# Moving the attention's keys and values by 64 bytes in a partition

## The reference

```python
scores = scale * np.matmul(q, k.transpose(0, 1, 3, 2))      # q, k, v: 4 x 8 heads x 576 x 64
scores = np.where(masks, scores, -1e9)                      # heads 0-3 local (32 back), 4-7 strided by 32
attn = softmax(scores)
x = (attn @ v), heads side by side                          # 2304 tokens x 512
h = x @ w_in; x = (h * sigmoid(1.702 * h)) @ w_out          # dense FFN, 512 -> 2048 -> 512
# then: tokens with x @ w_skip > 0 go to one of 8 experts (argmax of x @ w_gate),
# y = relu(x @ w1[e]) @ w2[e] (512 -> 1024 -> 512), out = x + gate * y; the others stay x
```

## The kernel before

| tile | bytes | address before | behind a multiple of 128 | of 256 |
|---|---|---|---|---|
| w_hi, w_lo, ident, gate_w | | 16512, 82048, 155776, 156800 | 0 | 128 |
| qs0, qs1 | 2304 | 165568, 167872 | 64 | 192 |
| ks0, ks1 | 2304 | 170176, 172480 | 64 | 192 |
| vs0, vs1 | 3072 | 174784, 177856 | 64 | 192 |
| probs0 to probs3 | 1536 | 180928 ... 185536 | 64 | 192 |
| probsT0, probsT1 | 1536 | 187456, 188992 | 64 | 64 |
| x_stage, x_hi, x_lo, g_hi, g_lo, x2, x2T | | 190528 and on | 64 | 64 |
| expert tiles read by TensorE (xg, xe, relu_h, h_hi, h_lo, h_rest) | | 164160 and on | 64 | 64 |

## Time and profile before

### The profile page before, as it was taken

The page is one execution under the profiler, slowest core; times in us unless marked ns, Lnnn a source line. Parts: engine busy times, 40 slices in busy tenths (PEclk is TensorE's granted clock), DMA queues, the critical chain, the costliest instruction groups (busy, mean ns, idle before and its releaser), DMA issues.

```text
span 700.0 us, 12990 instructions
## 1 busy us (share of the span) xinstructions
PE 654.6 (94%) x4457; PEld 560.1 (80%) x4458; DVE 392.2 (56%) x1374; ACT 356.4 (51%) x1025; POOL 156.1 (22%) x172
## 2 busy tenths in 40 slices
PE   3779999999999999999999999999998899998893
PEld 3568888888888889989899899898886687876772
DVE  4867774555445534334243343344658876878762
ACT  4878766655655533333333333334445665565650
POOL 5335421231223102001010010010114553213431
PEclk9989999999999999999999999999999999999897
DMA  7637634333421250201102002003346766577620
GB/s 243 202 126 249 216 105 161 100 95 109 132 74 40 79 168 1 91 1 31 61 1 90 0 0 90 0 1 106 91 136 179 251 223 214 178 250 246 212 93 14
DMA packets 45154, 81.53 MB, mean 116 GB/s; under 512 B 6594, under 2 KB 10690, under 8 KB 45088
## 3 DMA queue, kind: packets, MB, share of 16 engines
q1 hardware_dynamic: 41360, 75.01, 32.7%
q0 software_dynamic: 3184, 4.64, 2.1%
q10 hardware_dynamic: 544, 1.05, 0.4%
HBM read 65.06 MB, written 17.47 MB: 118 GB/s over the span
## 4 chain that ended last, share of the span: by engine, by line
PE 80%; DVE 5%; POOL 5%; DMA 3%; issue 3%; ACT 3%; POOLq 0%; DVEq 0%; ACTq 0%
PE ph L1440 28%; PE px L1453 28%; PE py L1573 5%; PE pe_h L1541 3%; PE pscore L1390 3%; PE ptrans L1399 3%; PE pctx L1412 2%; PE py L1577 2%; PE pe_h L1545 2%; DMA w_raw<-we 1%; DVE w_lo L1012 1%; PE phT L1557 1%; PE ph L1464 1%; POOL probs L689 1%; POOL slot_table L697 1%
## 5 line engine op out<-in xcount | busy, mean ns | idle before, releaser
L1440 PE MATMUL ph<-x_hi,w_hi 128*128 128x256 f32 x576 | 166.1, 288 | 1.0 <-DVE x_lo L1073 1.0
L1168 DVE SCALAR_TENSOR_TENSOR gated<-gated,ph 128x256 f32<-128x256 f32 x144 | 60.6, 421 | 187.7 <-ACT gated L902 186.4
L1440 PE MATMUL ph<-x_lo,w_hi 128*128 128x256 f32 x576 | 160.5, 279 | 0.0
L1440 PE MATMUL ph<-x_hi,w_lo 128*128 128x256 f32 x576 | 160.3, 278 | 0.0
L1453 PE MATMUL px<-w_hi,g_hi 128*128 128x512 f32 x288 | 117.7, 409 | 0.0
L1440 PEld LDWEIGHTS ph<-x_hi,w_hi 128*128 128x128 f32 x576 | 108.4, 188 | 8.2 <-issue 3.3
L1453 PE MATMUL px<-w_hi,g_lo 128*128 128x512 f32 x288 | 113.6, 394 | 0.0
L1453 PE MATMUL px<-w_lo,g_hi 128*128 128x512 f32 x288 | 113.0, 392 | 0.0
L1440 PEld LDWEIGHTS ph<-x_lo,w_hi 128*128 128x128 f32 x576 | 108.8, 189 | 3.6
L1440 PEld LDWEIGHTS ph<-x_hi,w_lo 128*128 128x128 f32 x576 | 108.7, 189 | 0.0
L902 ACT ACTIVATE gated<-ph 128x256 f32<-128x256 f32 x144 | 54.9, 381 | 102.3 <-PE ph L1440 99.3
(11 more groups left out here) (215 smaller groups left out, 1041.4 us busy)
## 6 DMA issues: line engine op xcount, KB each, us to landing
w_raw<-we SPq DMA_DIRECT2D x64, 256.0 KB, 2.9
more_raw<-we SPq DMA_DIRECT2D x64, 256.0 KB, 3.8
w_raw<-wf SPq DMA_DIRECT2D x32, 256.0 KB, 3.8
vs<-vw SPq DMA_DIRECT2D x16, 384.0 KB, 3.5
qs<-qT SPq DMA_DIRECT2D x16, 288.0 KB, 3.9
ks<-kT SPq DMA_DIRECT2D x16, 288.0 KB, 4.4
xT_dram<-x_stage SPq DMA_DIRECT2D x16, 288.0 KB, 3.3
x_lo<-xT_dram SPq DMA_DIRECT2D x8, 512.0 KB, 3.6
```

What stands on the lines that cost most here:

```text
L1168: nc.vector.scalar_tensor_tensor(gated[s % 2][:, :], gated[s % 2][:, :], 1.0, ph[s % 2][:, 0:TT], ALU.add, ALU.mult).then_inc(gated_done, 1)
L1440: last = nc.tensor.matmul(ph[f % 2][:, 0:TT], up_w(w, k, f), x[p][:, k, :], start=(at == 0 and n == 0), stop=(at == KD - 1 and n == 2))
```

## The change

Two tiles that nothing reads or writes are allocated, 64 bytes a partition each (16 float32): one between the queries and the keys, one between the values and the probabilities. Keys and values then begin at multiples of 128 bytes (ks0 at 170240, vs0 at 174848), and everything allocated behind the values moves by 128 bytes. Queries, masks, weights and the expert tiles stay where they are. No instruction is added or moved.

```diff
         qs = [sb(f"qs{i}", [P, S], to=ffn) for i in range(2)]
+
+        sb("gap_before_keys", [P, 16], to=ffn)
         ks = [sb(f"ks{i}", [P, S], to=ffn) for i in range(2)]
         vs = [sb(f"vs{i}", [P, 2, MAXBLK, D], to=ffn) for i in range(2)]
+        sb("gap_behind_values", [P, 16], to=ffn)
         probs = [sb(f"probs{i}", [P, MAXU, P], to=ffn) for i in range(SLOTS)]
```

## The result

The changed kernel takes 710.69 us (median of 4 runs, 706.74 to 711.85), the kernel before 702.8 in the same comparison (700.56 to 705.01). The ratio is 1.0088 with a 95% interval of 1.0052 to 1.0123: slower by 0.9%. The time lies above the forecast range, which ended at 706.7.

The account below looks back on a forecast made before the run. TensorE's own instructions were taken as the bound from 48 us through the dense stages. Attention -0.2, dense matmuls 0 and DMAs 0 gave 701.4 us for the profiled execution, 703.1 for the median, range 699.5 to 706.7.

Parts of the forecast that it names:

- What bounds the kernel: From 48 to 245 us and in the dense stage behind, TensorE's own instructions bound the kernel; before 48 us it waits.
- Scores and context: Attention's fp32 matmuls in the TensorE-bound stage: the changed address halves give -0.2 us, with -1.2 and +1.8 as ends.
- DMAs: Writes of keys and values: any alignment effect on the first keys, -0.5 to 0 us, would be hidden; price 0.
- The dense matmuls: Up and down matmuls, beside and dense stages: sequence entry, not place, picks the pace; price 0 us.
- the exchange of signs: Dense up and down swap their opposite-signed operand differences modulo 256; both cost alike per column, so price 0.
- The second rival: TensorE settles in its slower dense pace in both stages, x and g 192 behind 256: 8.5 us, 711.8; chance 0.07.
- The sum against the median: Whole kernel: -0.2 us on the profiled 701.6 gives 701.4; the runs' median, 703.3, is 1.7 higher, so forecast 703.1.

Follow-up runs that it names:

- the grid: A kernel of its own, not computing the reference: TensorE alone runs dense and score-like matmuls at varied operand places; up takes 113.3 ns at distance 64, 117.8 at 192.

## Why the prediction was wrong

- **What bounds the kernel**: right. The change's price was read where it was said to be, in TensorE's own pieces, and the waits did not move.
- **Scores and context**, -0.2 us with -1.2 and +1.8 as ends: right, and the truth was nearer 0. The nearest row, the transposes with their halves apart, told it: 0.90 and 0.72 us a group before and after, and no pair of places in the grid changes the form.
- **DMAs**, 0: right. Keys land after 4.5 us for 4.4, and nobody waits.
- **The dense matmuls**, 0: this is the step that failed, and two sentences of it. First, "the same operands at the same addresses have both paces, so what picks one is how the sequence enters, not where a tile lies". The first half of it holds: the entry counts, at either place. But that both paces exist at one place doesn't say that the place has no part. It sets how often the fast pace is reached: with x at 64 and g at 64, 82 of 92 up runs end at 113 ns a matmul, with both at 192 only 3 do, and with x at 64 and g at 128, 16. Second, the exchange of signs: up at distance 64 and down at 192 cost alike per column, from which I took the sign to be immaterial. Each form has its own good distance. Up is fast at 64 and slow at 192 (113.3 and 117.8 ns), down the other way round (233.4 and 228.9), so that exchanging the signs hits both. Two rows, each of one form at one distance, cannot show what either form costs at the other's. The dense steps, priced at 0, cost 5.3 us.
- **The second rival** was what happened, with a chance of 0.07. Its price of 8.5 us was too high: it took 1.42 us for either piece in both stages, and in the dense stage up has a mean of 1.41 and down of 1.40; the traces have 5.3 us in all. That the runs' median of 710.69 lies so near its 711.8 is partly luck, for 2.6 of the 7.9 us between the medians are not in the dense steps. Its condition, x and g 192 behind a multiple of 256, was the right one, and the trace of before held a hint: an excess of 7% that appeared only at the full clock, which the prediction itself laid to "two reading streams" and then priced at nothing for the very streams whose distance changed.
- **The sum against the median**: the profile of before was a low one of its kind (701.6, with medians of 703.1 over 28 later runs and 702.69 over 23 more), which the forecast allowed for.
- **The Trainium skill**, SBUF — State Buffer, "Who interferes with whom", has TensorE's two read ports independent and TensorE never waiting. The attention form agrees with it (0.82 us at 15 of 16 pairs of places). The dense forms don't: 113.3 and 117.8 ns for the same work at two distances, in a stretch of the grid kernel where no other engine of the core ran. There the measurement decides.

What makes the matmul wait is not shown. A collision of the two streams in the memory fits (it depends on the distance, and is gone at half the clock, where the earlier trace rows has 0.43 us for 512 columns, just what 512 cycles of 1.2 GHz take), but so far that is an argument. Why one and the same distance holds two paces is open too.

## What to carry to other kernels

A spacer that keeps the alignment modulo the number one believes in still moves everything behind it modulo the next power of two; look up which hot operands sit behind it before pricing it at nothing. Where TensorE is the bound, compare the start-to-start time of its commonest matmul before and after any change of layout: 2% there were 5.3 us here. And price an address that the trace has never seen with both ends open, or measure it on a grid of places first. Put the whole step into that grid: the one of single forms promised a gain for g at 128 that the sequence of both took back.

## What the runs showed of the hardware

The pace of a 128x128 by 256 matmul of the dense layer's kind varies between 113.3 and 123.5 ns at the 2.4 GHz level with the distance, modulo 256 bytes, between streamed operand and weights; that of a 512-column one between 226.7 and 240. The columns alone would take 107 and 213 by the half-clock rows (from 651.11 us on, nine matmuls of 512 columns start 3.84 us apart in all, 0.427 each). The distances that reach the best pace are few (two of 64 for up) and differ between the two forms; moving x and g by 256 bytes against the dense weights changed neither stage (241.1 and 235.1 us). One distance can hold two paces, 113 and 118 ns for up, and what ran before decides between them. So one form hands its state on to the next: down made 1.1 ns faster cost up 1.9 ns. fp32 matmuls of the attention's shape showed no dependence on the place (0.82 us a group at 15 of 16 pairs of places, 0.90 and 0.72 us in the kernel before and after).
